# Two expert networks behind a delta-rule attention on one core: token blocks of 512, transposed sums of the down products, the routing weight moved onto h

## What is computed

```python
def _attn_ref(q, k, v, beta):            # batch 4, heads 8, seq 768, head_dim 48
    k_n = k / (norm(k) + 1e-06)
    for t in range(S):
        y[t] = q[t] @ state
        state = state + beta[t] * outer(k_n[t], v[t] - state.T @ k_n[t])

def _moe_ref(x, w_gate, w1, w2):         # 3072 tokens, D 384, 8 experts, F 1024
    P = exp(x @ w_gate - max)
    for _ in range(8):
        P /= P.sum(1, keepdims=True) + 1e-09
        P /= P.sum(0, keepdims=True) + 1e-09
        P *= N / E
    for e in range(E):
        h = np.maximum(x @ w1[e], 0.0)
        out += P[:, e:e + 1] * (h @ w2[e])

def _moe2_ref(x, w_in, w_out):           # d_ff 2048
    h = x @ w_in
    return (h * sigmoid(1.702 * h)) @ w_out
```

## Time and profile before

| | |
|---|---|
| median of 3 runs | 2431.91 us (2430.31 to 2433.02) |
| the profiled execution | 2431.84 us |
| its span, first to last instruction | 2430.0 us |
| granted clock of TensorE, mean | 0.998 |
| PE busy, 17603 matmuls | 2387.9 us (98%) |
| DVE, ACT, POOL busy | 1001.4, 658.8, 823.1 us |

### The profile page before, as it was taken

One profiled execution on the slowest core, in us unless ns is written; L12 is line 12 of the kernel. 1 busy time (PEld: TensorE's weight loads), 2 busy tenths in 40 slices (PEclk: granted clock), 3 DMA queues, 4 the chain that ended last, 5 costly groups with the idle time before them and its releaser, 6 DMA issues.

```text
span 2430.0 us, 41927 instructions
## 1 busy us (share of the span) xinstructions
PE 2387.9 (98%) x17603; PEld 2325.6 (96%) x17603; DVE 1001.4 (41%) x2165; ACT 658.8 (27%) x1445; POOL 823.1 (34%) x831
## 2 busy tenths in 40 slices
PE   5999999999899999999999999999999999999999
PEld 4889989998899999999999999999999999999999
DVE  5876666663533333333333333333333333333332
ACT  3454444444211111111111111111111123222222
POOL 5654555442332233302311321230230413353432
PEclk9999999999999999999999999999999999999999
DMA  3243333322211012110110110111011100000001
GB/s 107 70 136 113 99 122 110 122 94 93 94 66 55 24 53 66 53 40 14 53 40 13 53 53 1 52 53 39 14 52 40 53 27 14 13 27 1 1 20 59
DMA packets 83963, 134.01 MB, mean 55 GB/s; under 512 B 5568, under 2 KB 62144, under 8 KB 83776
## 3 DMA queue, kind: packets, MB, share of 16 engines
q1 hardware_dynamic: 83776, 131.33, 16.5%
HBM read 98.28 MB, written 33.03 MB: 54 GB/s over the span
## 4 chain that ended last, share of the span: by engine, by line
PE 75%; DVE 1%; ACT 0%; issue 0%; ACTq 0%
PE bank L1393 41%; PE bank L1364 32%; PE bank L209 1%; PE bank L1340 0%; DVE rowsum L1585 0%; PE bank L1400 0%; PE bank L1291 0%; DVE route L1601 0%; PE bank L1283 0%; ACT L1445 0%; DVE route L1589 0%; DVE rowsum L1583 0%; ACT h_out L219 0%; DVE rowsum L1587 0%; DVE colsum L1593 0%
## 5 line engine op out<-in xcount | busy, mean ns | idle before, releaser
L1393 PE MATMUL bank<-w_hl,h_hl 128*128 128x384 f32 x5760 | 1018.2, 334 | 0.0
L1393 PEld LDWEIGHTS bank<-w_hl,h_hl 128*128 128x128 f32 x5760 | 1000.2, 188 | 0.0
L1364 PE MATMUL bank<-x_early,w_hl 128*128 128x384 f32 x3024 | 539.2, 334 | 0.7 <-ACT h_out L219 0.7
L1364 PEld LDWEIGHTS bank<-x_early,w_hl 128*128 128x128 f32 x3024 | 525.2, 188 | 1.0 <-issue 1.0
L1245 POOL TENSOR_TENSOR h_hl<-h_raw,h_hl 128x384 fp32r<-128x384 f32 x144 | 141.8, 1016 | 951.1 <-ACT h_hl L1463 951.1
L1471 ACT ACTIVATE h_hl<-bank 128x384 fp32r<-128x384 f32 x368 | 181.1, 492 | 907.6 <-PE bank L1364 907.6
L1536 DVE SCALAR_TENSOR_TENSOR h_hl<-bank,h_hl 128x384 fp32r<-128x384 f32 x368 | 205.3, 558 | 412.1 <-ACT h_hl L1471 412.1
L1558 DVE SCALAR_TENSOR_TENSOR x_sum<-bank,route,x_sum 128x384 f32<-128x384 f32 x288 | 178.0, 618 | 390.9 <-PE bank L1393 390.9
L209 PE MATMUL bank<-x_early,w_hl 128*128 128x384 f32 x1296 | 278.1, 352 | 0.0
L1364 PE MATMUL bank<-x_late,w_hl 128*128 128x384 f32 x1440 | 256.6, 334 | 0.0
L1364 PEld LDWEIGHTS bank<-x_late,w_hl 128*128 128x128 f32 x1440 | 250.1, 188 | 0.0
(11 more groups left out here) (125 smaller groups left out, 1889.7 us busy)
## 6 DMA issues: line engine op xcount, KB each, us to landing
w_raw<-in_moe_w SPq DMA_DIRECT2D x52, 768.0 KB, 6.3
h_early<-h_out SPq DMA_DIRECT2D x144, 192.0 KB, 1.9
h_raw<-h_early SPq DMA_DIRECT2D x36, 768.0 KB, 4.5
kq_t<-in_kq_rows SPq DMA_DIRECT2D x48, 256.0 KB, 2.7
kv<-in_kv_cols SPq DMA_DIRECT2D x24, 384.0 KB, 3.3
out<-x_sum SPq DMA_DIRECT2D x6, 576.0 KB, 3.0
w_raw<-in_moe_w_in SPq DMA_DIRECT2D x4, 768.0 KB, 4.3
w_raw<-in_moe_w_out SPq DMA_DIRECT2D x4, 768.0 KB, 4.5
```

The costliest lines, as they stand in the source:

```text
L1364: m = pe.matmul(bank[:, f, 0:TB], w1_hl[hn % 2][:, a, kc, f * P:(f + 1) * P], x_at(c, kc, b * TB, TB), start=n + kc == 0, stop=n == len(PA ...
L1393: m = pe.matmul(bank[:, 4 + t, 0:DM], h_hl[:, s % 2, a, f, t * P:(t + 1) * P], w2_hl[hn % 2][:, c, f, :], start=n + f == 0, stop=n == len( ...
```

## The change

`TB` becomes 512, so there are six blocks instead of eight, 120 units instead of 160, and 116 early items (29 units): 95 in the bodies 5 to 23, five a body, and 21 in the routing stretch. `x_early` holds 16 tiles instead of 18, and the last eight are turned in the routing stretch. `down` swaps its operands: `w2_hl` is stationary, h streams, and each of its three groups gives 128 outputs by 512 tokens. The sums so stay transposed; their parts are split by ACT and POOL where they lie (`next_high`, `next_low`), `turn_back` is gone, and the output leaves transposed. As a token is now a column, its weight can't be a scalar of a partition: `route` is transposed on PE, written to DRAM, and for each expert unit 512 weights are loaded to all partitions (`load_weight`). DVE makes relu times weight (`weighted`), ACT the high part, POOL the low part, for computed and loaded units alike, over two buffers. The first addend is copied, so nothing is zeroed.

```diff
-TB = 384
+TB = 512
-EARLY_FROM = 4
-UPS = 6
+EARLY_FROM = 5
+UPS = 5
...
-    later = [(hn, (1, 2)) for hn in range(4)]
-    return alone + both + later
+    return alone + both + [(0, (1,))]
...
-    ET = 18
+    ET = 16
...
+                def load_weight(s):
+
+                    hn, b = UNITS[s]
+                    wait(sp, dve_g, FC * (s - RING + 1))
+                    sp.dma_start(weight[:, s % RING, :].rearrange("p (t q) -> p t q", q=P),
+                                 route_dram[b * TT:(b + 1) * TT, hn // NH, :].unsqueeze(0).to_broadcast([P, TT, P])
+                                 ).then_inc(ld_r[s % RING], 16)
...
-                pool.memset(x_sum[:, :, :], 0.0)
...
-                pool.memset(x_last[:, :, :], 0.0).then_inc(pool_zero, 1)
                 high2(0)
                 low2(0)
...
+                for s in range(HALVES * NB):
+                    gated_low(s)
+                    if s - 2 in LAST_EXPERT:
+                        next_low(s - 2)
+                    hn, k = s // NB, s % NB
+                    if hn + 1 < HALVES:
+                        if k == 0:
+                            high1(hn + 1)
+                        elif k == 1:
+                            low1(hn + 1)
+                        elif k == 3:
+                            high2(hn + 1)
+                        elif k == 4:
+                            low2(hn + 1)
...
-                        if f == 0 and back is not None:
-                            turn_back(back)
...
-                                m = pe.matmul(bank[:, 4 + t, 0:DM], h_hl[:, s % 2, a, f, t * P:(t + 1) * P],
-                                              w2_hl[hn % 2][:, c, f, :], start=n + f == 0,
+                                m = pe.matmul(bank[:, 4 + kc, :], w2_hl[hn % 2][:, a, f, kc * P:(kc + 1) * P],
+                                              h_hl[:, s % 2, c, f, :], start=n + f == 0,
...
+                pe.wait_ge(dve_sink, 3 + 8 * SINKHORN)
+                for n, rows in enumerate(SPLIT_ROWS):
+                    pe.transpose(bank[0:rows.stop - rows.start, BR, n * P:(n + 1) * P],
+                                 route.rearrange("p t e -> p (t e)")[:, rows], ident[:, :]).then_inc(pe_rows, 1)
...
+                        wait(dve, pool_lo, n - 1)
+                        dve.scalar_tensor_tensor(out=gated[:, n % 2, :],
+                                                 in0=bank[:, f, :] if s in COMPUTED else h_raw[:, f, :], scalar=0.0,
+                                                 in1=weight[:, s % RING, :], op0=ALU.max, op1=ALU.mult
+                                                 ).then_inc(dve_g, 1)
...
-    out = nc.dram_tensor("out", (b * s, h * d), F32, kind="ExternalOutput").ap()
+    out = nc.dram_tensor("out", (h * d, b * s), F32, kind="ExternalOutput").ap()
```

More of the change, by code:

```diff
@@ L620, in body @@
-                        level(level_x, 5, 0)
                         chain(correct, 0)
                         level(level_y, 5, 1)
-                        early(43, 45)
+                        early(37, 45)
                         chain(correct, 1)
+                        level(level_x, 5, 0)
+                        level(level_x, 5, 1)
+                        chain(outputs, 0)
+                        level(level_y, 6, 1)
                         level(level_y, 6, 0)
-                        level(level_x, 5, 1)
@@ L685, in early @@
                                 early_w1_high(act, *split)
-                            if (item := slots(p)[UP_AT[k]]) is not None:
+                            if k < UPS and (item := slots(p)[UP_AT[k]]) is not None:
                                 early_relu(act, item[1], bank_of(item))
@@ L1043, in body @@
                             guarded(nrm)
+                        early(2)
                         if pre is not None:
@@ L1124, in build @@
         UNITS = [(hn, b) for hn in range(HALVES) for b in block_order(hn)]
-        AT = {unit: s for s, unit in enumerate(UNITS)}
-        COMPUTED = {unit: u for u, unit in enumerate(unit for unit in UNITS if not loaded(*unit))}
-        LOADED = {unit: n for n, unit in enumerate(unit for unit in UNITS if loaded(*unit))}
-        def back_at(s):
-            back = s - 1 - (FFN0 - 1) * NB
-            return back if 0 <= back < NB else None
+        COMPUTED = [s for s, unit in enumerate(UNITS) if not loaded(*unit)]
+        LOADED = [s for s, unit in enumerate(UNITS) if loaded(*unit)]
+        LAST_EXPERT = range((FFN0 - 1) * NB, FFN0 * NB)
         ROUTING = iter(range(IN_ATTENTION, EARLY))
-        BEFORE_MAX = [next(ROUTING) for _ in range(5)]
+        BEFORE_MAX = [next(ROUTING) for _ in range(4)]
         BEFORE_EXP = [next(ROUTING) for _ in range(3)]
@@ L1403, in _ @@
                         early(m)
-                up(*UNITS[0], None)
-                for s, unit in enumerate(UNITS):
-                    if s + 1 < len(UNITS) and not loaded(*UNITS[s + 1]):
-                        up(*UNITS[s + 1], back_at(s))
-                    down(*unit, back_at(s))
+                pe.wait_ge(act_exp, 1)
+                pe.wait_ge(dve_sink, 3 + 8 * SINKHORN)
+                for n, rows in enumerate(SPLIT_ROWS):
+                    pe.transpose(bank[0:rows.stop - rows.start, BR, n * P:(n + 1) * P],
+                                 route.rearrange("p t e -> p (t e)")[:, rows], ident[:, :]).then_inc(pe_rows, 1)
+                up(0)
+                for s in range(len(UNITS)):
+                    if s + 1 in COMPUTED:
+                        up(s + 1)
+                    down(s)
             @block.scalar
@@ L1506, in _ @@
+                gated_high(FC * HALVES * NB - 1)
             @block.vector
@@ L1603, in _ @@
                     dve.wait_ge(dve_sink, at + 8)
-                dve.wait_ge(pool_zero, 1)
-                relu_low(*UNITS[0], None)
-                for s, unit in enumerate(UNITS):
-                    if s + 1 < len(UNITS) and not loaded(*UNITS[s + 1]):
-                        if UNITS[s + 1][0] < FFN0:
-                            relu_low(*UNITS[s + 1], back_at(s))
-                        else:
-                            gate(*UNITS[s + 1], back_at(s))
-                    if unit[0] < FFN0:
-                        add_expert(*unit)
-                    else:
-                        add_quarter(*unit)
+                for n in range(RING):
+                    dve.wait_ge(st_h[n], 16 * len(range(n, EARLY, RING)))
+                weighted(0)
+                for s in range(len(UNITS)):
+                    if s + 1 < FFN0 * NB:
+                        weighted(s + 1)
+                    elif s + 1 < len(UNITS):
+                        gate(s + 1)
+                    add(s)
 def kernel(**inputs):
```

523 lines of the change are left out of this document (239 added, 284 removed).

## The result

| | before | after |
|---|---|---|
| median of 4 runs | 2431.35 us | 2386.51 us (2384.66 to 2387.11) |
| ratio, 95% interval | | 0.9814 [0.9802, 0.9826] |
| span of the profiled execution | 2430.0 us | 2384.8 us |
| mean granted clock of TensorE | 0.998 | 0.997 |

The change made the kernel 45 us faster. 2387 was predicted. The total hides errors of 5 to 6 us in either direction that cancel, so the terms matter more than the sum.

The account below looks back on a forecast made before the run. PE, issuing matmuls without a gap in the networks, was taken to bound the kernel, so time is their number by their pace. Terms summed to -45.0 us against 2431.84 us, giving 2387 us, range 2374 to 2425.

Parts of the forecast that it names:

- Pace: All fp32r matmuls: 8694 at 226.7 ns instead of 11592 at 173.3, the excess being a sum per matmul; -38.6 us.
- Rival B: Matmul excess is a share of the columns, so the pace term is 0; 2425 us, chance 0.17.
- Transposes: Between the networks: eight groups of nine PE transposes go, their replacement work on ACT and POOL covered; -7.2 us.
- Body 4: Attention: body 4 loses its early products, whose work stands elsewhere at full price; +4.6 us.
- Bodies: Attention: 19 other bodies have one piece less each, -1.6 us; the new order inside bodies adds no wait, 0.
- Rival C: The new attention bodies wait, 1 us in each of 24; 2411 us, chance 0.12.
- body 4 at 18: Sign to look for in attention: body 4, without early products, takes 18 us.
- 19 x 0.09: Attention: 19 bodies with one piece less each, a change of type costing 0.09 us; -1.6 us.
- Routing: Sinkhorn rounds: two rounds with one item wait 0.9 us each, +1.8; memsets go with their wait and half clock, -6.1 us.
- Start of the experts: Before the second `up`, PE waits for route weights stored to and loaded from DRAM; +2.1 us, bounds 0 and 7.
- Units: Expert units: each h passes DVE, ACT and POOL, covered by at least another `down`; cost 0, over 300 us without cover.
- Rival D: DVE and POOL exclude each other, delaying the 29 loaded units; 2491 us with POOL at 3.2 us, chance 0.06.

Follow-up runs that it names:

- experiment 1: Kernel after with added rows of fp32r matmuls (128 to 512 columns) and bf16 matmuls behind its last product, results unused; 2424.49 us in one run.
- Experiment 5: Kernel before with early products from body 5 on instead of body 4, six items moving to the routing stretch; 2437.02 us, ratio 1.0022.
- experiment 8: Kernel after with stored weights laid out by expert in DRAM, a block in one 2 KB piece instead of four of 512 B; 2383.07 us.
- Experiment 10: Kernel after with every low part of h made twice by POOL, first into a spare tile; 2413.61 us in one run.
- experiment 6: Kernel after with the first load of `w2` issued earlier, inside the Sinkhorn rounds; 2390.25 us, ratio 0.983 to the kernel before.
- experiment 7: Kernel after with the first load of `w2` issued behind the first load of weights; 2391.35 us, ratio 0.9834 to the kernel before.
- experiment 9: Kernel after with weights laid out by expert, the last early item behind the transposes of `route`, and its store ahead of the `w2` load; 2380.54 us.

## Why the prediction was right, step by step

- **Pace, -38.6 us: right.** The excess is a sum per matmul (226.5 ns in the stretch, 226.7 from row to row), and experiment 1 shows that also at 256 and 320 columns. Rival B falls.
- **Transposes, -7.2 us: right**, 8.0 measured; the reading left out the 0.09 us behind each nine. `next_high` and `next_low` are covered.
- **Body 4, +4.6 us: right.** Experiment 5 has 4.5.
- **Bodies: right.** The first solve of body 5 stands at 136.03, so the bodies from 5 to 23 take (580.05 - 136.03) / 18 = 24.67 us each, where 24.7 to 24.9 was said. Rival C falls; the empty bodies even gained 0.6 us in three. The sign "body 4 at 18" can't be read from first solves: from that of body 4 to that of body 5 are 20.4 us, as 18 early matmuls of body 5 already stand between them. A slip of 0.1: 19 x 0.09 is 1.7, not 1.6.
- **Routing, +1.8 - 6.1 us: right in place, off by pieces.** The rounds with one item wait 0.5 us, not 0.9, so their cost is 1.0. The 3.6 us of waiting that I gave to the memset were 2.0 from it and 1.6 from the splits. Those went as well, because the longer rounds cover them, and with them 1.6 us in the third round that the prediction did not count.
- **Start of the experts, +2.1 us: wrong in size,** 5.1 of waiting and 2.6 at the lower clock in the profiled execution, 7.7 in all. That is above its bound of 7; the three other traces of this code have 6.0 to 7.4. The step that failed is the times of the way through DRAM: "the route behind it at about 6.5, the first weights at 9.5". They were 6.6 (the load's issue, 657.68) and 12.8. So the failing number is the load's 3.0 us, taken from a DMA of as many bytes: in pieces of 512 B it was 6.2 us here, and 3.4 in pieces of 2 KB (experiment 8). The lower clock behind the wait stood in the upper bound but not in the sum; behind the 2.00 us of experiment 8, a wait as long as the one forecast, there is none. The time of the store came out right, though not by its working, in which it needs only 1.4 us behind `w2`: it landed 4.1 and 5.2 us after its issue. That was luck.
- **Units, 0: right,** with room. No `down` waits. Experiment 10 shows how much: POOL's low parts twice cost 27 us, not the hundreds that a chain without cover would.
- **Rival D** was not idle: the exclusion lengthens one operation in each of the 29 loaded units by 1.1 us (1.76 against 0.68), some 30 us of DVE, all under PE. Its price of 2491 needed POOL at 2.7 us for a low part; it is 1.29.

The errors cancel, and two stretches show where. From the first `up` of the experts on (645.49 before, 651.10 after) the profiled executions differ by 50.8 us, and the terms with what was measured give it: 50.3 of pace and 8.0 of transposes less 7.7 at the start of the experts, 50.6. Ahead of it the kernel after is 5.6 us longer, where the terms of attention and routing, with their part of the pace, add up to 10.5. Of these 4.9 us, the wait in the third round is 1.6, the rounds with one item 0.8, the empty bodies 0.6. The other 1.9 us I can't assign. That they nearly make up for the start of the experts (5.6 more than said) is luck: the total came out right to 0.5 us, its parts did not.

## What to carry to other kernels

Where PE is issued without a gap, count its matmuls and price what each has over its columns: in fp32r that was 13.3 ns, so a quarter fewer and wider matmuls for the same columns were worth 1.6% here. A value that turns around through DRAM needs a store and a load that each take several microseconds before anyone may use it; give them work to hide under on the waiting engine, and make each partition's piece one long run. And a wait put down to one cause may have two: take one away by itself before the whole wait is booked to it.

## What the runs showed of the hardware

- fp32r matmuls with 128 by 128 weights have 13 ns or a little more over their columns from 256 columns on, and a floor of 111.7 ns at 128 and 192; bf16 ones have 2.5 ns at 128 to 512 (experiment 1). Between 400 and 512 columns the value of fp32r is up to 7 ns higher in the probes, which is not explained.
- A load of 256 KB to 128 partitions took 4.9 us in pieces of 512 B and 3.2 us in pieces of 2 KB (medians of 96 each).
- A store of 32 KB landed 4.9 and 5.2 us after its issue where a load of 768 KB was issued just ahead of it (experiment 8 and the kernel after), and 3.4, 4.0 and 1.8 us where none was (experiments 6, 7 and 9). Why these three differ is open.
- Behind waits of PE of 2.7 to 5.2 us in the routing and the networks the matmuls nearly always ran at the lower clock level, at a cost of 1.6 to 3.0 us each by the rows of 18 and 36 matmuls behind them; behind one of 3.5 us (experiment 6) they did not, nor behind any of 1.2 to 2.1 us. The length of the wait does not decide alone: in experiment 10 the level fell once behind an idle time of 0.67 us.
- POOL and DVE shut each other out for a whole instruction in some forms of DVE's work. An operation on two tiles of SBUF, 0.68 us alone, took 1.76 us beside a low part of POOL in 29 of 29 cases, and a `TENSOR_SCALAR` of 24 columns on one tile, 0.18 us alone, took 0.77 to 3.23. Operations that read a PSUM bank kept their time (211 of 211 of the `weighted` ones), and so did `TENSOR_REDUCE` on a tile of SBUF (0.35 us both ways).
